# Delta rule and two feed-forward layers on one core: TensorE's tile loop without the products into `warm_ps`

## The reference

```python
k_n = k / (norm(k) + 1e-06)
for t in range(S):                       # per batch and head, state is 48 x 48
    y[:, :, t] = einsum('bhd,bhde->bhe', q[:, :, t], state)
    v_old = einsum('bhde,bhd->bhe', state, kt)
    state = state + bt * einsum('bhd,bhe->bhde', kt, vt - v_old)
# then, on x = y reordered to (3072, 384):
h = x @ w_in;  g = P(h) / (Q(h) + 1e-06);   x = g @ w_out      # layer 1
h = x @ w_in2; g = h * tanh(softplus(h));   out = g @ w_out2   # layer 2
```

## Time and profile before

| | |
|---|---|
| median of 3 runs | 1280.1 us (1276.27 to 1285.77) |
| the profiled execution | 1278.46 us, its span 1276.6 us |
| TensorE busy / weight loads | 1160.3 us (91%) / 891.4 us (70%) |
| VectorE, ScalarE, GpSimd busy | 933.3, 742.7, 194.8 us |
| delta rule, first to last pass | 72.8 to 427.3 us of the span |
| products into `warm_ps` from `eye` | 348, of which 336 in the 48 passes |

### The profile page before, as it was taken

One profiled execution on the slowest core, in us unless ns is written; L12 is line 12 of the kernel. 1 busy time (PEld: TensorE's weight loads), 2 busy tenths in 40 slices (PEclk: granted clock), 3 DMA queues, 4 the chain that ended last, 5 costly groups with the idle time before them and its releaser, 6 DMA issues.

```text
span 1276.6 us, 23607 instructions
## 1 busy us (share of the span) xinstructions
PE 1160.3 (91%) x9612; PEld 891.4 (70%) x9612; DVE 933.3 (73%) x1042; ACT 742.7 (58%) x956; POOL 194.8 (15%) x365
## 2 busy tenths in 40 slices
PE   6169798979999888999999999989999999999998
PEld 3146465757666666777778777777788888888886
DVE  2733344334444499999999999999978788888776
ACT  1123333332434486777777777777766676767664
POOL 1518465546730000000000000000000000000000
PEclk7567796778899999999999999989999999999999
DMA  6973756373544210101001010213100010101000
GB/s 145 213 158 91 153 129 157 85 166 77 139 112 138 63 50 1 50 1 49 1 0 49 0 50 1 99 50 100 49 26 25 14 36 0 50 0 50 1 26 25
DMA packets 81727, 83.83 MB, mean 66 GB/s; under 512 B 55072, under 2 KB 62752, under 8 KB 81056
## 3 DMA queue, kind: packets, MB, share of 16 engines
q1 hardware_dynamic: 70912, 60.43, 18.7%
q10 hardware_dynamic: 10720, 22.03, 6.2%
HBM read 61.99 MB, written 20.45 MB: 65 GB/s over the span
## 4 chain that ended last, share of the span: by engine, by line
DVE 32%; PE 29%; issue 3%; ACT 2%; DVEq 0%; ACTq 0%
PE o_ps L828 5%; PE o_ps L830 5%; PE o_ps L829 5%; PE h_ps L828 5%; PE h_ps L830 5%; PE h_ps L829 5%; DVE val L1045 5%; DVE val L1013 5%; DVE val L1032 5%; DVE g_lo L1051 4%; DVE den L1005 4%; DVE den L1040 4%; DVE pa L1011 4%; DVE w_lo_late L87 0%; DVE den L1042 0%
## 5 line engine op out<-in xcount | busy, mean ns | idle before, releaser
L901 ACT ACTIVATE g_hi<-val 128x1024 fp32r<-128x1024 f32 x96 | 102.0, 1062 | 102.1 <-DVE val L1045 96.1
L828 PE MATMUL o_ps<-g_hi,w_hi_late 128*128 128x512 f32 x288 | 117.1, 407 | 19.7 <-DVE g_lo L1051 19.7
L681 DVE TENSOR_TENSOR u_blk<-hz_ps,w_blk 128x768 f32<-128x768 f32 x48 | 46.0, 958 | 119.4 <-PE hz_ps L390 119.4
L525 ACT ACTIVATE stage<-y_ps 128x256 f32<-128x256 f32 x48 | 18.2, 380 | 188.8 <-PE y_ps L422 188.5
L828 PE MATMUL o_ps<-g_hi,w_hi_early 128*128 128x512 f32 x288 | 114.5, 398 | 14.8 <-ACT stage L938 9.3
L1045 DVE SCALAR_TENSOR_TENSOR val<-den,val 128x1024 f32<-128x1024 f32 x96 | 117.7, 1226 | 10.7 <-DVE den L1040 0.5
L1051 DVE SCALAR_TENSOR_TENSOR g_lo<-val,g_hi 128x1024 fp32r<-128x1024 f32 x96 | 117.7, 1226 | 1.6 <-ACT g_hi L901 1.5
L367 PE MATMUL warm_ps<-eye 128*128 128x512 bf16 x348 | 115.9, 434 | 0.0
L828 PE MATMUL h_ps<-x_hi,w_hi_early 128*128 128x512 f32 x288 | 112.4, 390 | 2.4 <-DVE val L1013 2.0
L829 PE MATMUL o_ps<-g_lo,w_hi_late 128*128 128x512 f32 x288 | 114.2, 396 | 0.0
L828 PE MATMUL h_ps<-x_hi,w_hi_late 128*128 128x512 f32 x288 | 112.6, 391 | 1.6 <-DVE w_lo_late L87 1.6
(11 more groups left out here) (97 smaller groups left out, 2387.2 us busy)
## 6 DMA issues: line engine op xcount, KB each, us to landing
w_raw<-w SPq DMA_DIRECT2D x14, 768.0 KB, 4.5
kq_gram<-kq_t SPq DMA_DIRECT2D x12, 768.0 KB, 11.1
x_raw<-x_dram SPq DMA_DIRECT2D x12, 768.0 KB, 5.7
kq_run<-kq_t ACTq DMA_DIRECT2D x40, 192.0 KB, 4.0
kv_run<-kv_n ACTq DMA_DIRECT2D x20, 384.0 KB, 5.0
k_norm<-kv_n SPq DMA_DIRECT2D x6, 768.0 KB, 5.2
x_dram<-stage ACTq DMA_DIRECT2D x24, 192.0 KB, 4.7
x_dram<-stage SPq DMA_DIRECT2D x6, 768.0 KB, 4.3
```

The source lines that it names most:

```text
L828: nc.tensor.matmul(dst, hi, rhs_hi, start=first, stop=False)
L901: act_fn(g_hi[:, n % 2], val[:, n % 2], ACT.Copy, scale=-1.0).then_inc(g_hi_ready, 1)
```

## The change

In `tile` of TensorE the three calls of `keep_warm` go, 7 products in each of the 48 passes, 336 in all. Those ahead of the loop and in `feed_forward` stay. Nothing else changes, no wait and no other instruction; all that follows moves up by three lines.

```diff
                         if gram and FIRST_FILL <= G2 * c + g < FIRST_FILL + 4:
                             gram_fill(tau + 2, G2 * c + g - FIRST_FILL)
-                        keep_warm(4)
                         solve(tau, c, g)
-                        keep_warm(2)
                         q_state(tau, c, g)
-                        keep_warm(1)
                         update(tau, c, g)
                         before = (c, g)
```

## The result

| | before | after |
|---|---|---|
| median | 1282.4 us (1273.11 to 1290.59, 20 runs) | 1295.6 us (1281.38 to 1304.35, 20 runs) |
| profiled execution, span | 1276.6 us | 1301.8 us |
| first `k_state` to last `within` | 354.5 us (72.80 to 427.33) | 377.4 us (72.75 to 450.14) |

The ratio is 1.0106, with a 95% interval of 1.0077 to 1.0135: slower by 1.1%. The prediction was 1293.0, in a range of 1270 to 1304. Some executions of a kernel are slower than the others, among them the profiled one of the kernel after (1303.67 us); the medians here are of all executions, the ratios leave the slow ones out. So the profiled pair lies 25 us apart and the medians 13. A second profile of the same kernel (1300.24 us) ended its last `within` at 446.60 us, and its passes have the same lengths.

What follows compares the result with a forecast made beforehand. TensorE's stream bounds the tiles, its clock level setting their cost. At 0.50 nearly throughout, tiles add 8.5 us, seams 3 and `feed_forward` entry 3: 14.5 on the profiled execution's 1278.46 gives 1293.0 us, range 1270 to 1304.

Steps and rivals of the forecast that it cites:

- The level decides: Tiles 1 to 5: without the products TensorE's granted clock falls to 0.50 to 0.60; low level nearly throughout, 1286 to 1300, chance 0.52.
- The mark for being wrong: Over the tiles: the forecast fails if passes of 3.7 to 5.3 us make up more than a tenth.
- third rival: Tiles: TensorE's high level holds and GpSimd's inverses set the tiles, 1238 us; high level for over 20% of passes, chance 0.10.
- rule of the Trainium skill: TensorE: matmuls stay at the fast level while they follow each other without a long wait for a transfer; would give 1238.
- A product's price: Each pass at 0.50: removing seven products saves 3.21 us, leaving 8.33 us with a Gram part and 6.47 without.
- seams: Small gaps ahead of `solve` and `update` where products stood: 0 to 0.1 us a pass, 0 to 5 us, taken as 3.
- The wait for `z`: Ahead of `solve`: `within` covers VectorE's answer at 0.50, so at most 0.1 us a pass, no idle over 0.2 us.
- Tiles 0 and 1: Tile 1 begins at 145, its `solve` between 146.0 and 149.8 (taken 147); the following restart takes 3.6 us.
- chain of inverses: Between tiles: next `solve` at least 26.1 us after Gram parts are stored; that wait hides behind the restart, under 1 us.
- The entry to `feed_forward`: Start of `feed_forward`: entered at 0.50, twelve products take 5.1 us instead of 3.01; bounds 0 and 6, taken as 3.
- the level comes back often enough: Tiles: high level returns for 5 to 20% of the passes, giving 1266 to 1286 us; chance 0.30.
- Worse than the sum: Tiles and entry: unhidden `x_blk` waits, seams and entry at upper bounds, restarts 2 us longer: 1305; above 1300, chance 0.08.

Runs made afterwards that it cites:

- thin run: Kernel before, with all seven products of each pass using 32x32 of the array instead of 128x128, same 512 columns: 1446.1 us, ratio 1.1173.
- seven everywhere: Kernel before, with all seven products of every pass placed together ahead of `solve` instead of 4, 2 and 1: 1252.5 us, ratio 0.9661.

## Why the prediction was right, and where its sum was not

**The level decides.** Right. Over tiles 1 to 5 I wrote 0.50 to 0.60; it was 0.64, 0.50, 0.53, 0.53, 0.50, so tile 1 lies outside. The mark for being wrong, more than a tenth of the tiles at the high level, was just not passed (0.10 and 0.08). The thin run shows the cause, with the same queue and no level. The third rival (the high level holds, 1238) did not come about, and the trace speaks against the rule of the Trainium skill behind it as I had read it: from 222.92 to 264 us TensorE was busy for 40.97 of 41.08 us, and the clock is 0.50. (The rule: "TensorE: Matmul & The Clock Gate", section "Loop structure matters more than you think".)

**A product's price.** This is the larger of two terms that were mis-sized. I took 3.21 us for the seven of a pass from start to start, and forecast passes of 8.33 and 6.47 us. They take 8.61 and 6.75. What goes with seven products is 11.54 - 8.61 = 2.93, or 0.42 us for each: the rest, 0.28 us, belonged to the groups beside them and stayed. Over 48 passes that is 13 us, against which I had set 3 for seams. With it my sum for the last `within`, 435.8, becomes 449.2; it ended at 450.14 in one profile and at 446.60 in the other, both beyond my 435 to 441. That 449.2 comes so near is itself a balance, of the waits for `z` and the tile starts against the level coming back, below. By tiles, the sum was short by 5.2, 4.4, 4.0 and 5.0 us in tiles 2 to 5, and 4.3 too long up to the start of tile 2 (209.3 against 204.96).

**The level coming back.** My sum had none. In the two profiles the share was 0.10 and 0.08, and it saved what the passes cost more, in part. How much it saves differs from run to run: the 20 runs spread over 23 us. So the misses stand against each other, and that the median came out 2.6 us from the forecast is in part luck: both profiled executions, where the terms can be read, took 5.6 and 8.1 us more than the median of their runs. By how much a median execution's tiles were shorter no trace shows.

**The wait for `z`.** This is the other mis-sized term: I had bounded it by 0.1 us a pass, 0 to 5 us in all, since `within` would cover VectorE's answer, and forecast no idle row over 0.2 us in a pass. In pass 7 of every tile but tile 3, in pass 3 of tiles 4 and 5 and in pass 1 of tiles 1 to 3 TensorE waits 0.62 to 1.71 us, and in pass 0 of every tile but tile 2 0.60 to 0.75. From the waits of the kernel after in 72 to 450 us:

```profile
PE hz_ps L390 <- DVE z L670: 14.2, 15, 1.7
...
PE hz_ps L390 <- DMA x_blk<-inv_dram: 2.0, 1, 2.0
```

That is 14.2 us in 15 places, where the kernel before had 5.4 in 8. It is not all new time, since the four products that stood there took 1.7 us at the low level. But in those passes removing the products gives back less than their length.

**Tiles 0 and 1.** SP's queue and TensorE at the restart ahead of tile 1, after the change:

```profile
132.72 0.36 SPq L273 DMA_DIRECT2D inv_dram<-inv_x  x1
...
138.28 10.56 SPq L283 DMA_DIRECT2D x_blk<-inv_dram  x16
```

```profile
142.59 0.57 PE L379 MATMUL ks_ps<-state,kq_run 48*32 48x48 f32 x32 [1.64 <-issue]
143.86 1.91 PE L390 MATMUL hz_ps<-z,x_blk 128*128 128x48 f32 x8 [0.70 <-DVE z L670]
```

Tile 1's `solve` could begin at 143.86, before my 146.0 to 149.8. The restart was idle for 1.64 us there and for 4.51 and 2.45 ahead of tiles 2 and 3, where I had taken 3.6 each time (before: 5.60, 3.60 and 4.49), and the `x_blk` issue was at 138.28 instead of 143.49: the keys' load was issued 4 us earlier, and the store of the inverse landed 5.6 us after its issue at 132.72. The load being out of its way is my reading; the store ahead of tile 2 had the keys issued 1.8 us before it and took 14 us as before. That part of the sum was too high by 3 us. In this profile the chain of inverses bounds only tile 2: `solve` waited 2.0 us for `x_blk` there, over the 1 us that I had set as the mark for being wrong, and not in tile 3. In the second profile such a wait, of 2.73 us, stands in tile 1 and none in tiles 2 and 3, so the chain lies close to TensorE's own path in either.

**The entry to `feed_forward`.** From the timeline of TensorE after:

```profile
451.88 5.46 PE L869 MATMUL h_ps<-w_hi_early 128*128 128x512 f32 x12 [1.74 <-PEq L112]
457.14 0.57 PE L825 MATMUL h_ps<-x_hi,w_hi_early 128*128 128x512 f32 x1
```

The twelve products took 5.3 us to the next row, as forecast (5.1). The level was back at 457.5, by their end, and the hidden products then follow at about 0.24 us each (457.55 to 457.79 in the trace). `feed_forward` is 2.4 us longer in all; I had 3.

**Other rivals.** That the level comes back often enough to make no change, 0.30, did not happen in the median, though the two fastest of the twenty (1281.4 and 1282.2) are such runs. *Worse than the sum* was nearer than its 0.08: 4 of the 20 took more than 1300 us, and the profiled execution, 1303.7, lies near 1305 with other terms than those I named.

## What to carry to other kernels

Work that only keeps TensorE busy is to be judged by the granted clock of the window, not by its busy time: here it costs 0.42 us a product at the low level and pays by nearly halving everything beside it (a pass with Gram part takes 11.54 us at 0.50, and 183.01 - 176.66 = 6.35 at 1.00, both in the kernel before). Put it in one piece, where TensorE waits for another engine anyway: there it brings the level back and removes the idle time behind which the level was lost. Moving the seven products ahead of `solve` was worth 3%, moving them behind `q_state` cost 1%, and taking them all out cost about 1%. More of them where a restart or a transfer lets the level fall left 4 short stretches at 0.50 where there were 7, without a time that is clear of seven everywhere. When a removed group's price is read from start to start, part of that length belongs to its neighbours and stays.

## What the runs showed of the hardware

- 336 matmuls of 32x32 weights, each of the same length as those of 128x128, left the granted clock at 0.51 over 521 us, with TensorE busy for 504 of them. The same number with 128x128 weights gave 0.84 over 355 us.
- `solve` (four float32 matmuls of 128x128 weights and 48 columns) takes 1.58 us between long 128x128 products, 1.72 between short ones and 1.87 up to `q_state` without either, at 0.50. Between 32x32 products of the same length as the long ones it takes 1.87 too, and its first weight load does not begin ahead of its first matmul there (284.07 both), where it begins 0.43 us ahead behind a 128x128 product. At 1.00 it is 0.83 behind a product and in front of one (184.80 to 185.63 in the kernel before), and 1.02 without (176.39 to 177.41 in the kernel after).
- The restart of TensorE's loop was idle for between 1.64 us (after) and 6.48 us (seven ahead), in kernels that differ only in their products.
